# Moving the weighing and key products ahead in VectorE's order, in a fused attention, SoLU and expert kernel

## The reference

```python
scale = np.minimum(mag, 0.999) / (mag + 1e-06)
a_re_n, a_im_n = (a_re * scale, a_im * scale)
for t in range(S):
    ar, ai = (a_re_n[:, :, t, :, None], a_im_n[:, :, t, :, None])
    new_re = ar * S_re - ai * S_im
    new_im = ar * S_im + ai * S_re
    kv = np.einsum('bhd,bhe->bhde', k[:, :, t], v[:, :, t])
    S_re, S_im = (new_re + kv, new_im)
    y[:, :, t] = np.einsum('bhd,bhde->bhe', q[:, :, t], S_re)
```

## Time and profile before

| | us |
|---|---|
| time before, median of 3 executions | 1375.03 |
| lowest and highest of them | 1373.91, 1377.15 |
| the profiled execution, its own time | 1372.84 |
| span of its instructions in the trace | 1371.1 |
| first phase's loop over tiles, in the trace | about 73 to 810 |
| TensorE busy, whole span | 1131.7 |
| VectorE busy, whole span | 869.5 |

### The profile page before, as it was taken

One profiled execution on the slowest core, in us unless ns is written; L12 is line 12 of the kernel. 1 busy time (PEld: TensorE's weight loads), 2 busy tenths in 40 slices (PEclk: granted clock), 3 DMA queues, 4 the chain that ended last, 5 costly groups with the idle time before them and its releaser, 6 DMA issues. The chain is left out here.

```text
span 1371.1 us, 21866 instructions
## 1 busy us (share of the span) xinstructions
PE 1131.7 (83%) x7864; PEld 983.6 (72%) x7864; DVE 869.5 (63%) x1715; ACT 621.1 (45%) x964; POOL 444.6 (32%) x416
## 2 busy tenths in 40 slices
PE   0017789978887997798999539999999999999996
PEld 0015566655665665576777539999999999999996
DVE  4758548838854864884343247777777777777772
ACT  5241453454346345343333235555555555555551
POOL 3020131214223233221324232444444444444432
PEclk9967879989988998898999759999999999999998
DMA  9210031021013001011110066667667776666650
GB/s 273 85 66 18 18 87 47 24 50 61 24 32 103 24 24 41 24 47 36 31 47 18 12 230 210 238 234 243 232 224 251 252 251 235 223 229 223 230 189 1
DMA packets 85979, 167.50 MB, mean 122 GB/s; under 512 B 18566, under 2 KB 57696, under 8 KB 85872
## 3 DMA queue, kind: packets, MB, share of 16 engines
q1 hardware_dynamic: 72432, 137.71, 31.5%
q0 software_dynamic: 13440, 28.40, 5.8%
HBM read 148.83 MB, written 21.92 MB: 125 GB/s over the span
## 5 line engine op out<-in xcount | busy, mean ns | idle before, releaser
L1302 PE MATMUL bank<-sxh,w1h 128*128 128x256 f32 x744 | 212.2, 285 | 1.9 <-DVE sxl L1248 1.9
L1302 PE MATMUL bank<-sxh,w1l 128*128 128x256 f32 x744 | 210.5, 283 | 0.0
L854 ACT ACTIVATE hh<-bank 128x256 fp32r<-128x256 f32 x248 | 95.2, 384 | 253.9 <-PE bank L1302 253.9
L1302 PE MATMUL bank<-sxl,w1h 128*128 128x256 f32 x744 | 210.2, 283 | 0.0
L1271 DVE SCALAR_TENSOR_TENSOR hl<-bank,hh 128x256 fp32r<-128x256 f32 x248 | 104.7, 422 | 117.4 <-ACT hh L854 117.4
L646 POOL DMA_INDIRECT out<-yo,mine x62 | 78.0, 1258 | 276.4 <-DVE yo L1264 267.0
L1488 PE MATMUL bank<-w2h,hh 128*128 128x384 f32 x496 | 167.5, 338 | 0.0
L1488 PE MATMUL bank<-w2l,hh 128*128 128x384 f32 x496 | 166.7, 336 | 0.0
L1488 PE MATMUL bank<-w2h,hl 128*128 128x384 f32 x496 | 166.5, 336 | 0.0
L1293 PE MATMUL bank<-ident,kp 128*128 128x128 f32 x160 | 34.1, 383 | 145.4 <-DVE kp L1035 145.4
L1302 PEld LDWEIGHTS bank<-sxh,w1h 128*128 128x128 f32 x744 | 140.6, 189 | 2.3 <-DVE sxl L1248 2.3
(11 more groups left out here) (183 smaller groups left out, 2628.9 us busy)
## 6 DMA issues: line engine op xcount, KB each, us to landing
raw<-in_w SPq DMA_DIRECT2D x62, 1536.0 KB, 7.0
ar<-in_a_re SPq DMA_DIRECT2D x6, 768.0 KB, 4.7
turn<-in_a_im SPq DMA_DIRECT2D x6, 768.0 KB, 6.0
qk<-in_q SPq DMA_DIRECT2D x48, 96.0 KB, 2.4
qk<-in_k SPq DMA_DIRECT2D x48, 96.0 KB, 2.5
out<-wide SPq DMA_DIRECT2D x9, 512.0 KB, 12.2
vt<-in_v SPq DMA_DIRECT2D x24, 192.0 KB, 2.7
xs<-x SPq DMA_DIRECT2D x24, 192.0 KB, 2.8
```

Of the source, the lines that this page charges most:

```text
L854: nc.scalar.activation(hh[:, f % NH, :], bank[:, f % 2, 0:CAP], ACT.Relu).then_inc(hh_done, 1)
L1302: ins = MM(dst, stationary[a_](cc), moving[b_](cc), start=(n_ == 0), stop=(n_ == len(terms) - 1))
```

## The change

Only VectorE's list is written in another order; no instruction is added or removed. `weigh` and `k_products` of tile n now stand right behind the addition to the state, ahead of the last running products and of `xl`. `q_products` stands behind `xl` as before. Both `newton` of round 3, and the first `norm` of round 0, move behind `q_products`.

```diff
                                     bank[:, 6, 0:2 * NP * D], ALU.add).then_inc(w_added, 1)
+                if has(n):
+                    weigh(n)
+                    k_products(n)
                 fill(share - made[0])
-                if b == 0 and prep and c > 0:
-                    norm(2 * c + 2)
                 if has(m):
                     dve.wait_ge(xt_hi, m + 1)
                     wait(dve, h_mm, m)
                     V.tensor_tensor(xl[0:PR]...
-                if b == 3 and prep:
-                    newton(2 * c + 2)
-                    newton(2 * c + 3)
                 if has(n):
-                    weigh(n)
-                    k_products(n)
                     q_products(n)
                 if n == 0:
                     weights_rest(0)
                     weights_rest(1)
-                    norm(2)
+                if b == 3 and prep:
+                    newton(2 * c + 2)
+                    newton(2 * c + 3)
                 if b == 0 and prep:
+                    norm(2 * c + 2)
                     norm(2 * c + 3)
```

## The result

The changed kernel takes **1351.62 us** (median of 4 runs, 1346.20 to 1364.06) against 1374.47 for the kernel before (4 runs, 1372.51 to 1377.15): ratio 0.9846, 95% interval 0.9814 to 0.9879. That is 22.9 us less; the forecast was 1350.5. What strikes at once is the spread: 18 us between the changed kernel's runs, under 5 between the four of before. The profiled execution took 1354.94 us, its span 1353.2. Where lines are named, those of the changed kernel behind the edit are one lower than before in TensorE's part (the score block is L1349, the transposes L1292) and one higher for `xl` (L1184).

The account below looks back on a forecast made before the run. It took a ring in the loop (y, xh, xl, weighing, kp, transposes) as the bound. 2.3 + 17.2 + 8.5 + 8.2 - 18.0 + 6.4 = 24.6 us off 1375.03 gave 1350.5 us; range 1335 to 1366.

Parts of the forecast that it names:

- The gains: All savings in the loop before the clock's loss is taken off: 42.6 us.
- round 3 into 0: Five passages into round 0: kp wait goes, zl becomes the bound, 1.0 us earlier in four, 8.5 us in all.
- the fifth case: Last chunk's passage from round 3 into round 0, with no squares behind it: zl comes 4.5 us earlier.
- The last chunk: No transposes of kp there; four waits for zl of 1.5 to 1.8 us each all go: 6.4 us.
- The clock: Nine score blocks behind new idle time run at low clock, losing 2.0 us each: -18.0 us.
- The upper bound of 6.1: Most a score block could lose to the clock, the whole block at half clock: 6.1 us each.
- the case called slower: All nine score blocks wholly at 1.2 GHz lose 55 us together against the gains: 1387 us, chance 0.05.
- The collision: Round 0: Newton's third and fourth instruction meet GpSimd's two additions, costing 3.5 us in each of four cases.
- The rival in which GpSimd gives way: No collision of Newton with GpSimd's additions in round 0: 14 us more gained, 1336.5 us, chance 0.16.
- Rounds 1 and 2: Weighing and kp run in VectorE's wait for xh; four pairs of rounds gain 4.3 us each, 17.2 in all.
- the third rival: VectorE becomes the bound in rounds 1 and 2; pairs give 8.2 instead of 17.2 us: 1359.5 us, chance 0.18.
- Newton and `norm`: Moving the first norm back costs nothing beside; qp and norm meeting L534 in another order costs at most 1.6 us.

Follow-up runs that it names:

- Kernel 10: Kernel before with only weighing and key products moved up, plus 28, 16 and 18 added matmuls ahead of the score block: 1323.86 us.
- kernel 3: Changed kernel with ScalarE's four squares of round 0 moved behind zh, kt and the state's copies: 1351.57 us.
- kernel 6: Changed kernel with ScalarE's squares behind the state's copies and waiting for zl, no added matmuls: 1339.40 us.
- kernel 5: kernel 4 with ScalarE's squares behind the state's copies and waiting for zl, and 16 instead of 30 added matmuls in round 0: 1315.28 us.
- kernel 4: Changed kernel with unused matmuls filling TensorE's wait for zl ahead of the score block in nine places: 1327.95 us.
- kernel 8: Kernel before with 28, 17, 7 and 7 added matmuls ahead of the transposes of kp: 1383.34 us.
- kernel 9: Kernel before with added matmuls ahead of the transposes of kp and ahead of the score block: 1368.43 us.

## Why the prediction was right, and where its terms were off

**The mechanism.** The marks it named are there: 3.1 us of wait for `kp` (forecast: under 10), 54.4 us for `zl` in nine tiles (some 50), `xl` of round 2 without a wait behind L947, L998 and L1002 over 2 us beside L530, and `zl` behind VectorE's own list. One is there in part: the `xh` waits fell by 21.5 us, 1.2 per wait and not 2. Kernel 10 shows that `kp` early is the whole gain.

**The gains, 42.6 forecast.** Medians give 1374.5 - 1328.0 = 46.5 with the clock's losses filled away, 3.9 more, and 49 if the overrun of the filling is added. By the table the largest difference is round 3 into 0, where the fifth case gave the 4.5 forecast and the four others 3.1 and three times 1.6 instead of 1.0. In the three, VectorE's way from the end of `xl` to the end of `zl` is 392.93 to 403.57, 10.6 us, not 11.3. In the first case the gate's small instructions are not yet there, and the way is 9.3 us. The last chunk gave 8.3 instead of 6.4, because before the last score block itself took 7.6 us at a lower clock, which the four waits alone did not say.

**The clock, -18.0 forecast.** This term was mis-sized: 1351.6 - 1328.0 = 23.7 by the medians, 2.6 per place instead of 2.0 (about 26 and 2.9 with the overrun of the filling), and 3.3 per place in the profiled execution. The 2.0 was taken from 5.7 us behind the long `kp` wait. The score block of 6.05 us stands behind waits of 4.6 to 7.7, and in three places it ran nearly whole at half clock (0.52, 10.5 us). The largest loss was 4.5. The upper bound of 6.1 was wrong in itself, as it takes a block at half clock to last twice as long. Kernels 3 and 6 have one such block each, and it takes 10.7 us; the one of kernel 3 (body 16):

```profile
516.40:527.10 10.70, 10.70 (x46) 7.27 (x48) 1.12 (x1) 0.00 (x0) 0.00 (x0) 0.50 0.09 19
```

Nine times 4.7 make 42, no more than the gains: by the score blocks alone, the case called slower could at worst have come out even. The two errors, 3.9 and 5.7, nearly cancel; that the forecast came within 1.1 us of the median is in good part luck, the more so as the changed kernel's four runs differ by 18 us, where the prediction took 2.8 us for measurable. The Trainium skill, "TensorE: Matmul & The Clock Gate", section "HAM oscillation — how this bites in real kernels", tells of a gap that comes back in every pass and slows the start of each. The trace agrees in all nine places: the granted clock of the blocks was 0.52 to 0.74.

**The collision, 3.5 in four chunks forecast.** 3.1 in the timeline, 3.2 by kernel 5. The rival in which GpSimd gives way and VectorE loses nothing is refuted, though GpSimd loses too (4.29 us for the pair instead of 3.61). The Trainium skill, "SBUF — State Buffer", section "Who interferes with whom", says that a VectorE instruction with two inputs in SBUF contends with a GpSimd instruction that reads SBUF. The trace agrees: L998 and L1002 took 2.58 and 2.44 us instead of 0.95.

**Rounds 1 and 2.** 4.3 per pair forecast, 4.7 measured. VectorE is the bound of `xl` in round 2, as reckoned, but the pair gives more than the 2.05 of the third rival.

**Newton and `norm`.** Moving the first `norm` back was costed at nothing, and its meeting with L534 at up to 1.6 us. That meeting ended instead: L983 takes 1.36 us in the mean of eight in kernel 10, without the late moves, and 0.54 in the changed kernel, while Newton's pair collides only there. Net, by the end of `zl` in kernels 4 and 10, the late moves neither bring nor cost time.

## What to carry to other kernels

Before moving work off a ring, write down what stands behind the next wait on the same engine: here 72 us of wait for `kp` became 42 us more of wait for `zl`, and the clock's loss moved from a place with slack to one without. To learn what an order is worth, fill the long waits of both kernels with matmuls nobody reads and compare these (here 40.5 us); the difference to the plain kernels is the clock (6 us before, 24 after), and filling may be worth keeping in itself. Differences of a few us need one more look: how far the filling runs over the wait, and which waits were left unfilled. And place what another engine's output starts (squares, then GpSimd's sums) by whose list it will meet, not by when its input is ready.

## What was not expected of the hardware

- The loss at low clock varies for the same wait: behind 7.68 and 7.69 us the score block took 7.9 us once and 10.5 twice, behind 5.1 us from 9.1 to 10.5. The changed kernel's runs differ by 18 us, and by 3.1 once the waits are filled; the kernel before, whose long waits are those for `kp`, ranged from 1369.48 to 1380.25 in 20 runs.
- Short waits can bring the clock down as well: in kernel 8 blocks behind waits of 2.7 and 3.1 us took 7.6 to 10.5 us, in kernel 9 one behind 1.52 us took 9.07, while others behind the same wait took 6.05.
- A GpSimd addition of 1.83 us holds small instructions up too: L1083 on 64 elements took 1.44 us. And GpSimd pays: its two additions took 4.29 us (changed kernel) and 4.50 (kernel 3) together with VectorE in between, 3.61 in kernel 5 without it.
